# The first expert slot fed from ten early tiles and two late ones, the last projection and the first head in halves

## The chip, the cores and the metric

The kernel runs on one core of a Trainium2 chip, in one launch. The metric is device time in microseconds (us), and lower is better. Every run of the kernel before lies between 775.5 and 778.18 us, with 776.9 us in the middle of three.

## The reference

Three stages follow each other. Only the shapes and the steps that the change touches are kept here.

```python
# 1 attention: B=2, H=8, S=768, D=64
q_bits = (q @ proj > 0); k_bits = (k @ proj > 0)      # proj: 64 x 6
mask = bucket(q_bits)[:, None] == bucket(k_bits)[None, :]
attn = softmax(where(mask, q @ k.T / 8, -1e9)); attn_out = attn @ v
x = attn_out -> (1536, 512)
# 2 gated layer, 512 -> 1536 -> 512
xn = x / sqrt(mean(x*x) + 1e-6) * rms_g
x = (silu(xn @ w_gate) * (xn @ w_val)) @ w_out
# 3 eight experts, each token goes to one
e_idx = argmax(x @ gate_w); weight = softmax(x @ gate_w)[e_idx] * sigmoid(x @ out_gate)[e_idx]
for e in range(8):
    rows = x[e_idx == e]
    out[e_idx == e] = weight * (relu(rows @ w1[e]) @ w2[e])      # 512 -> 1024 -> 512
```

## The kernel before

There are five engines: PE (matrix products), ACT, DVE and POOL (elementwise work) and SP (which only starts transfers). Each follows its own hand-written list and waits on semaphores. Nearly every product is made of three, from operands split into a high and a low part (names that end in `_h` and `_l`), so an operand is first converted (high, mostly ACT) and then subtracted (low, mostly DVE).

**Attention** takes the 16 heads in 8 pairs. A pair is a `period` of 12 steps. A step makes one score tile of 128 queries by 768 keys on PE (`scores`), its row maximum on DVE (`maxes`, L1442) and its exponential on ACT (`exps`, L1199). After three steps DVE inverts the sums (`denoms`, L1452 and L1454), POOL multiplies the three tiles by them (L710) and PE turns the tiles (`turn`, L899), five steps behind the scores. Pair 0 has no predecessor that prepares it. Its keys and queries come in eight transfers (`load_first` on SP and L1278 on ACT), ACT converts them (`first_highs`, L1173; `own_queries`, L1177), DVE makes the low parts of its first head (L1571) and POOL those of its second head (`second_lows`, L614), and PE projects both heads onto the six directions in halves of the sequence, numbered `m` = 0 to 3 (`project_first`, L865). PE passes the first microseconds with 36 products whose results nobody reads (`keep_warm`, L977), and makes two further groups of eight of them in period 0.

**The gated layer** makes all 12 tiles (128 tokens each) of the hidden values and then, tile after tile, `project(tt)` on PE: 36 products of 512 columns into a bank of PSUM (L1086). ACT scales the result into `x2` (L1320). PE turns `x2` and multiplies it with the router's weights (`turn_x2`, L1068; `gate_logits`, L1076), DVE chooses the expert (`choose`, L1673 to L1683), PE counts the token's place among those of its expert (`ranks`, L1059), DVE makes the row number `dest` (`put`, L1688 to L1696), and POOL scatters the 128 rows of the tile to the DRAM tensor `routed`, which is ordered by expert (L821). In PE's list the routing of tile `tt` stands between the products of the next two tiles.

**The experts** are eight slots, each up to 256 rows. A slot needs its rows (`rows_in`), turned on PE (`turn_rows`, L1120), in high and low part (`rowsT`, L1349; `low_rowsT`, L1745), and the expert's weights, which come in four pieces of 1 MB (`load_piece`) and are split by ACT and DVE (`split_piece`, L1338 and L1626). Then `up` makes 96 products of 256 columns (L1134), ACT and DVE split the hidden values (L1354, L1751), and `down` makes two halves of 24 products of 512 columns (L1146). The rows of the next slot are loaded and turned meanwhile. The first slot has nobody before it: SP waits until all twelve scatters have landed (L579) and only then loads `rows_in[0]`. PE makes 36 idle products between the count and `turn_rows(0)`, and ten more between that and `up`.

```python
sp.wait_ge(scattered, 16 * NT)                                         # L579
sp.dma_start(rows_in[0][:], blocks_v[:, first_block(0)]).then_inc(rows_loaded[0], 16)
```

Of the kernel before, what the change touches and what calls it, by code (L numbers as in the profile page):

```python
# [11 lines left out]
I32 = mybir.dt.int32  # L12
# [10 lines left out]
FIRST_PROJ_STEP = 5  # L23

# [8 lines left out]
def build(nc, q, k, v, proj, w_gate, w_val, w_out, rms_g, router, out_gate, w1, w2, out):  # L33
# [46 lines left out]
    with ExitStack() as ctx:  # L80
# [27 lines left out]
        logits = at("logits", [P128, NT, 2 * E], F32)  # L108
# [19 lines left out]
        dest_f = at("dest_f", [P128, NT], F32)  # L128
        dest = at("dest", [P128, NT], I32)
        count_f = at("count_f", [1, E], F32)  # L130
# [93 lines left out]
        DVE_LOWS = ([(1, c) for c in range(C)] + [(tg, c) for tg in (2, 3) for c in range(C)])  # L224
        addr[0] = x2_offset
# [29 lines left out]
        for i in range(3):  # L255
# [17 lines left out]
                 "alone_put exp_done denom_done rden_ready norm_done turned high_ready low_ready pv_done "  # L273
# [3 lines left out]
                 "x2_turned x2T_made logits_made logits_out best_made flag_made before_made z_made route_step route_exp ranks_made counted placed "  # L277
                 "table_made scattered w1_high w2_high w1_low w2_low rows_turned rowsT_high rowsT_low hid_made "
# [5 lines left out]
         alone_put, exp_done, denom_done, rden_ready, norm_done, turned, high_ready, low_ready, pv_done,  # L284
# [3 lines left out]
         x2_turned, x2T_made, logits_made, logits_out, best_made, flag_made, before_made, z_made, route_step, route_exp,  # L288
         ranks_made, counted, placed,
         table_made, scattered, w1_high, w2_high, w1_low, w2_low, rows_turned, rowsT_high, rowsT_low, hid_made,  # L290
# [13 lines left out]
        rows_loaded = [sem(f"rows_loaded{i}") for i in range(2)]  # L304
        rows_stored = [sem(f"rows_stored{i}") for i in range(2)]
# [65 lines left out]
        row_banks = (ps_t[0], ps_o)  # L371
        out_banks = (ps_t[1], ps_p)
# [55 lines left out]
        def _(sp):  # L428
# [53 lines left out]
            def load_first(r, halves):  # L482
                for w, src in ((KEYS, k_v), (QUERIES, q_v)):
                    for half in halves:
                        sp.dma_start(first_raw[lanes(half), w, r], src[0, r]).then_inc(first_in[2 * r + w], 16)

            load_first(0, (0,))
            load_first(1, (0, 1))
# [10 lines left out]
            sp.wait_ge(cleared, 6)  # L499
# [88 lines left out]
        def _(pool):  # L588
# [178 lines left out]
            for n, rows in enumerate((k_b[0], k_b[1], q_b[1])):  # L767
                for r in range(2):
                    wait(pool, cleared, 2 * n + r)
                    nc.gpsimd.memset(rows[lanes(1 - r), r].bitcast(F32), 0.0).then_inc(cleared, 1)  # L770
# [1040 lines left out]
```

## Time and profile before

| | us |
|---|---|
| median of three runs | 776.9 |
| the profiled run, as timed | 776.07 |
| its span, first to last instruction | 774.3 |
| PE busy within the span | 754.2 |
| attention, to about | 245 |
| gated layer: hidden values, to about | 450 |
| gated layer: projection and routing, to about | 565 |
| from the last projection to the first expert product | 565.4 to 581.3 |
| eight slots | 581.3 to 769 |

The profile is one execution. Its clock starts at the first instruction. Where PE is busy without a break its work is the time, whatever the others do. Where PE stands, the view of waits names what it stood for, and the chain of waits shows, backwards from the last instruction, which step released which. The time as timed is 1.8 us above the span; that part lies around the kernel.

### The profile page before, as it was taken

How to read it: one execution, taken by the hardware profiler on the slowest of the kernel's cores; microseconds unless marked ns; L12 is line 12 of the kernel's file. 1: busy time of each engine (PE TensorE's matmuls, PEld its weight loads, DVE VectorE, ACT ScalarE, POOL GpSimd, SP SyncE). 2: the span in 40 equal slices, each digit the busy share in tenths (PEclk: the TensorE clock that was granted, in tenths of full speed). 3: DMA queues.
4: the chain of work that ended last, by engine and by line, in shares of the span. 5: the costliest groups of instructions: out<-in, count | busy, mean ns of one | idle time of the engine just before them, and what ended most of it. 6: DMA issues, size and time to landing. Idle time of an engine off the chain costs nothing.

```text
span 774.3 us, 13374 instructions
## 1 busy us (share of the span) xinstructions
PE 754.2 (97%) x4562; PEld 688.4 (89%) x4562; DVE 476.7 (62%) x930; ACT 377.1 (49%) x671; POOL 313.0 (40%) x345
## 2 busy tenths in 40 slices
PE   7999999999999999999999999999979999999996
PEld 6789899888888999999999988888869998899995
DVE  6999999999987654334334344455554554565430
ACT  5888889888887311111111133534333444455431
POOL 7977877789788573333443001211210011000111
PEclk9999999999999999999999999999999999999999
DMA  7897679659501222111110040022352656765400
GB/s 205 216 271 212 191 202 231 191 137 239 133 10 44 78 76 63 41 41 41 41 52 29 0 164 25 21 84 76 137 184 87 229 193 223 254 217 197 157 25 23
DMA packets 54011, 97.53 MB, mean 126 GB/s; under 512 B 6761, under 2 KB 21109, under 8 KB 53960
## 3 DMA queue, kind: packets, MB, share of 16 engines
q1 hardware_dynamic: 49496, 86.48, 38.1%
q0 software_dynamic: 2240, 6.31, 2.1%
q10 hardware_dynamic: 2224, 4.08, 1.9%
q8 instruction: 30, 0.49, 0.3%
q14 instruction: 21, 0.17, 0.1%
HBM read 58.25 MB, written 22.10 MB: 104 GB/s over the span
## 4 chain that ended last, share of the span: by engine, by line
PE 83%; DVE 9%; issue 3%; ACT 2%; DMA 2%; POOL 1%; ACTq 0%; POOLq 0%; DVEq 0%
PE ps_t L1086 13%; PE ps_s L946 13%; PE ps_s L1134 12%; PE ps_t L946 6%; PE ps_t L899 6%; PE ps_t L1146 6%; PE ps_p L1146 6%; DVE pT_l L1460 4%; PE ps_o L946 3%; PE ps_p L946 3%; PE ps_s L885 3%; DVE negmax L1442 3%; PE ps_s L886 3%; PE ps_o L914 1%; PE ps_o L916 1%
## 5 line engine op out<-in xcount | busy, mean ns | idle before, releaser
L710 POOL TENSOR_SCALAR probs<-probs,rden,alone 128x768 f32<-128x768 f32 x96 | 93.9, 992 | 33.8 <-DVE rden L1454 33.7
L1460 DVE TENSOR_TENSOR pT_l<-ps_t,pT_h 128x384 fp32r<-128x384 f32 x192 | 97.6, 549 | 5.8 <-ACT pT_h L1209 4.7
L946 PE MATMUL ps_s<-xn,w_h 128*128 128x384 f32 x384 | 97.5, 334 | 0.0
L1199 ACT ACTIVATE probs<-ps_s,negmax 128x768 f32<-128x768 f32 x96 | 87.2, 908 | 17.5 <-DVE negmax L1442 16.9
L1209 ACT ACTIVATE pT_h<-ps_t 128x384 fp32r<-128x384 f32 x192 | 85.4, 492 | 16.6 <-PE ps_t L899 15.3
L1442 DVE TENSOR_REDUCE negmax<-ps_s 128x1 f32<-128x770 f32 x96 | 91.0, 948 | 4.0 <-PE ps_s L886 3.1
L1134 PE MATMUL ps_s<-rowsT_h,expert_w 128*128 128x256 f32 x512 | 92.4, 281 | 0.6 <-DVE rowsT_l L1745 0.6
L899 PE MATMUL ps_t<-ident,probs 128*128 128x128 f32 x576 | 87.4, 282 | 4.6 <-DVE pT_l L1460 2.7
L827 POOL DMA_INDIRECT out_dram<-rows_out,rows_in x16 | 15.8, 986 | 182.2 <-ACT rows_out L1360 182.2
L899 PEld LDWEIGHTS ps_t<-ident,probs 128*128 128x128 f32 x576 | 63.0, 140 | 24.4 <-DVE pT_l L1460 10.2
L1626 DVE TENSOR_TENSOR expert_w<-piece,expert_w 128x2048 fp32r<-128x2048 f32 x32 | 72.6, 2291 | 15.4 <-ACT expert_w L1338 15.1
L1134 PEld LDWEIGHTS ps_s<-rowsT_h,expert_w 128*128 128x128 f32 x512 | 79.1, 189 | 1.1 <-issue 0.8
L821 POOL DMA_INDIRECT routed<-x,dest x12 | 21.1, 1758 | 128.2 <-DVE x L1695 128.2
L1134 PE MATMUL ps_s<-rowsT_l,expert_w 128*128 128x256 f32 x256 | 71.9, 281 | 0.0
L946 PEld LDWEIGHTS ps_s<-xn,w_h 128*128 128x128 f32 x384 | 69.4, 188 | 0.0
L885 PE MATMUL ps_s<-k_a,q_a 128*128 128x384 f32 x192 | 65.1, 339 | 1.9 <-ACT probs L1199 1.0
L1751 DVE SCALAR_TENSOR_TENSOR hidT_l<-ps_s,hidT_h 128x512 fp32r<-128x512 f32 x32 | 22.1, 689 | 71.3 <-ACT hidT_h L1354 71.3
L886 PE MATMUL ps_s<-k_b,q_b 128*128 128x384 f32 x192 | 64.8, 337 | 0.0
L946 PE MATMUL ps_s<-xn,w_l 128*128 128x384 f32 x192 | 64.1, 334 | 0.0
L1338 ACT ACTIVATE expert_w<-piece 128x2048 fp32r<-128x2048 f32 x32 | 60.2, 1908 | 0.0
L1086 PE MATMUL ps_t<-wo_h,hs_h 128*128 128x512 f32 x144 | 59.2, 411 | 0.0
L1086 PE MATMUL ps_t<-wo_h,hs_l 128*128 128x512 f32 x144 | 56.4, 392 | 0.0
(243 smaller groups left out, 1695.5 us busy)
## 6 DMA issues: line engine op xcount, KB each, us to landing
piece<-in_moe_w_dram SPq DMA_DIRECT2D x32, 1024.0 KB, 6.3
routed<-filler SPq DMA_DIRECT2D x56, 257.0 KB, 4.6
k_a<-qk_h SPq DMA_DIRECT2D x28, 192.0 KB
rows_in<-routed ACTq DMA_DIRECT2D x7, 514.0 KB, 3.7
rawv<-in_v_dram SPq DMA_DIRECT2D x8, 384.0 KB, 5.9
w_raw<-in_moe_w_gate_dram SPq DMA_DIRECT2D x12, 256.0 KB, 3.1
w_raw<-in_moe_w_val_dram SPq DMA_DIRECT2D x12, 256.0 KB, 3.4
wo_raw<-in_moe_w_out_dram SPq DMA_DIRECT2D x12, 256.0 KB, 2.6
```

Source lines behind the costliest of these rows:

```text
L710: nc.gpsimd.tensor_scalar(pr, pr, rden[:, j:j + 1], alone[:, j:j + 1], ALU.mult, ALU.add).then_inc(norm_done, 1)
L885: nc.tensor.matmul(o, q_a[par][:, r, queries], k_a[par][:, r, keys], start=True, stop=False)
L886: mm = nc.tensor.matmul(o, q_b[par][:, r, queries], k_b[par][:, r, keys], start=False, stop=True)
L899: mm = nc.tensor.transpose(ps_t[kt % 2][:, i * P128:(i + 1) * P128], probs[:, 3 * g + i, kt * P128:(kt + 1) * P128], ident[:])
L946: mm = nc.tensor.matmul(unit_banks[tg][w][:, 0:G], a_[par][:, w, c, :], xn_at(tg, part, c), start=(n == 0), stop=(n == 3 * C - 1))
L1086: mm = nc.tensor.matmul(ps_t[par][:], a_[par][:, f, :], b_[:, f, :], start=(f == 0 and n == 0), stop=(f == NF - 1 and n == 2))
L1134: mm = nc.tensor.matmul(hid_banks[b][:, i * ROWS:(i + 1) * ROWS], a_[:, side, c, f:f + P128], b_[:, c, :], start=(n == 0), stop=(n == 3 * ...
L1146: mm = nc.tensor.matmul(out_banks[half][:], a_[:, c, half_cols(half)], b_[:, side, c, :], start=(c == 0 and t == 0), stop=(c == CF - 1 and ...
L1199: nc.scalar.activation(probs[:, j].rearrange("p (a n) -> p a n", a=2), third(ps_s[j % 2]), ACT.Exp, bias=negmax[:, j:j + 1], accum_out=psu ...
L1209: nc.scalar.activation(pT_h[u % 4][:], ps_t[kt % 2][:, 0:G], ACT.Copy).then_inc(high_ready, 1)
L1442: nc.vector.tensor_reduce(negmax[:, c], with_floor(ps_s[j % 2]), AX.XY, ALU.max, negate=True).then_inc(max_done, 1)
L1460: nc.vector.tensor_tensor(pT_l[u % 4][:], ps_t[kt % 2][:, 0:G], pT_h[u % 4][:].bitcast(F32), ALU.subtract).then_inc(low_ready, 1)
```

## The change

It has three parts and some waits that belong to them.

**The hand-over to the first slot.** SP loads the 512 data columns of `rows_in[0]` after ten scatters (`early_rows_in`). The last two columns of each row (the output row and the factor) are loaded once all twelve have landed. The scatter of tile 10 waits for the early load. PE multiplies the early rows with the unit matrix into two cleared banks (`turn_early`, eight products) instead of turning them. The rows of tiles 10 and 11 are added to these banks by 16 products of 256 columns: the tile's high and low part times a matrix of ones and zeros (`onehot`), which has a one where a token goes to a place among the first 256 (`add_late`). `up` of every slot now takes the eight products with the high rows first and the four with the low rows after them. The 58 idle products around the hand-over are gone.

**The last projection in halves.** `project(11)` is made for the left 256 columns and then for the right ones, with the router's work for the left half between them. `ranks(tt-1)` moves to the end of `project(tt)`. `choose` reads PSUM directly.

**The first head in halves.** The transfers of pair 0 are in another order. The low part of the first head's queries is made in two halves, and the fourth projection (`m` = 3) comes behind the first scores. Four clears move from POOL to DVE and five small writes of `proj_w` from DVE to POOL. ACT normalises the third tile of pair 0 and makes `own_queries(1)` later, the first `denoms` stands ahead of the fourth `maxes`, and the two groups of eight idle products become groups of four. DVE's `denoms` and POOL's `put_alone` of all later periods wait for `first_norm`, too.

```diff
 sp.wait_ge(first_in[KEYS], 32)          # new, between the loads of head 0 and of head 1
...
-            sp.wait_ge(scattered, 16 * NT)
-            sp.dma_start(rows_in[0][:], blocks_v[:, first_block(0)]).then_inc(rows_loaded[0], 16)
+            sp.wait_ge(scattered, 16 * (NT - LATE))
+            sp.dma_start(rows_in[0][:, :, 0:DM], blocks_v[:, first_block(0), :, 0:DM]).then_inc(early_rows_in, 16)
+            sp.wait_ge(late_scattered, 16 * LATE)
+            sp.dma_start(rows_in[0][:, :, DM:DM + 2], blocks_v[:, first_block(0), :, DM:DM + 2],
+                         allow_slow_non_contiguous=True).then_inc(rows_loaded[0], 16)
...
+                if tt == NT - LATE:
+                    pool.wait_ge(early_rows_in, 16)
...
             for tt in range(NT):
                 project(tt)
+            project(NT - 1, 1)
+            def turn_early(first, last):
+                pe.wait_ge(early_rows_in, 16)
+                pe.wait_ge(banks_cleared, 1)
+                for n in range(first, last):
+                    c, half = divmod(n, 2)
+                    nc.tensor.matmul(place_in_first(c)[:, half_cols(half)], rows_in[0][:, half, c * P128:(c + 1) * P128],
+                                     ident[:], start=(half == 0 and c % 2 == 0), stop=False)
+            def add_late(i):
+                pe.wait_ge(onehot_made, i + 1)
+                pe.wait_ge(late_low, (1, 3)[i])
+                for c in range(C):
+                    for part in (late_h, late_l):
+                        mm = nc.tensor.matmul(place_in_first(c), part[i][:, c * P128:(c + 1) * P128], onehot[i][:],
+                                              start=False, stop=(i == LATE - 1 and c % 2 == 1 and part is late_l))
...
-                step(nc.vector.tensor_reduce(one(dest_f, tt), chosen[:], AX.X, ALU.add))
-                nc.vector.tensor_copy(one(dest, tt), one(dest_f, tt))
+                    step(nc.vector.tensor_reduce(one(dest_f, i), chosen[:], AX.X, ALU.max))
+                    nc.vector.tensor_scalar(onehot[i][:], slot_f[:], one(dest_f, i), None,
+                                            ALU.is_equal).then_inc(onehot_made, 1)
...
+                        if j == 2:
+                            own_queries(1)
+                        if j == 3:
+                            act.wait_ge(rden_ready, 1)
+                            act.wait_ge(alone_put, 1)
+                            nc.scalar.activation(probs[:, 2], probs[:, 2], ACT.Identity, bias=alone[:, 2:3],
+                                                 scale=rden[:, 2:3]).then_inc(first_norm, 1)
-                        if j in (0, 2, 3):
-                            high_ahead(1, 1, max(0, j - 1))
+                        if j in (0, 3, 4):
+                            high_ahead(1, 1, max(0, j - 2))
...
                 wait(dve, norm_done, 3 * (n - 4))
+                if not (isinstance(P, int) and P == 0):
+                    dve.wait_ge(first_norm, 1)
```

PE's list before, from the end of the last projection to the first expert product. `x_174` is `x2`, `ps_o` the bank for turned tiles, `ps_p` that of the router, and the products `ps_t<-ident` and `ps_s<-ident` with no second operand are the idle ones.

```order
L1076 MATMUL ps_p<-gates,x2T_178 128x16 [waits logits_out,x2T_made]
L1076 MATMUL ps_p<-gates,x2T_178 128x16 x3
L977 MATMUL ps_s<-ident 128x128 x6
L1059 MATMUL ps_s<-flag_b,before_b 128x8 [waits flag_made]
L1060 MATMUL ps_s<-before_tile_b,ones_b 128x8
L977 MATMUL ps_s<-ident 128x128 x6
L1112 MATMUL ps_s<-before_tile_b,ones_b 128x8 [waits before_made]
L1113 MATMUL ps_s<-neg_base_b,ones_b 128x8
L977 MATMUL ps_s<-ident 128x128 x36
L1120 MATMUL ps_t<-ident,rows_in_180 128x128 [waits rows_loaded0]
L1120 MATMUL ps_t<-ident,rows_in_180 128x128 x3
```

The same place after the change:

```order
L1130 MATMUL ps_p<-gates,x2T_188 128x16 [waits x2T_left,z_made]
L1130 MATMUL ps_p<-gates,x2T_188 128x16
L1112 MATMUL ps_o<-ident,x_184 128x128 [waits x2_made,x2T_made]
L1112 MATMUL ps_o<-ident,x_184 128x128
L1177 MATMUL ps_t<-ident,rows_in_190 128x128 [waits banks_cleared,early_rows_in]
L1177 MATMUL ps_t<-ident,rows_in_190 128x128
L1130 MATMUL ps_p<-gates,x2T_188 128x16 [waits x2T_made,z_made]
L1130 MATMUL ps_p<-gates,x2T_188 128x16
...
L1103 MATMUL ps_s<-flag_b,before_b 128x8 [waits flag_made]
...
L1185 MATMUL ps_t<-onehot_179,late_h_176 128x256 [waits late_low,onehot_made]
```

The idle products have gone, two of the four router products stand ahead of the right half's turning, and the load of the early rows is waited for in front of the other two.

ACT's list before, from the start to the first turned tile of pair 0 (`k_a`, `q_b` and `q_a` are the operands of the scores, `qk_h` and `raw` belong to the next pair, `pT_h` is the turned tile):

```order
L1173 ACTIVATE k_a_103<-first_raw,lane_scale 128x768 [waits first_in2]
L1173 ACTIVATE q_b_106<-first_raw,lane_scale 128x768 [waits first_in3]
L1177 ACTIVATE q_a_105<-first_raw 64x768
L1199 ACTIVATE probs,psums<-ps_s,negmax 128x768 [waits max_done]
L1189 ACTIVATE qk_h_100<-raw_112 128x768 [waits qk_in1]
L1199 ACTIVATE probs,psums<-ps_s,negmax 128x768 [waits max_done] x2
L1189 ACTIVATE qk_h_100<-raw_112 128x768
L1199 ACTIVATE probs,psums<-ps_s,negmax 128x768 [waits max_done]
L1189 ACTIVATE raw_112<-raw_112 128x768
L1199 ACTIVATE probs,psums<-ps_s,negmax 128x768 [waits max_done]
L1209 ACTIVATE pT_h_119<-ps_t 128x384 [waits turned]
```

And after:

```order
L1264 ACTIVATE k_a_103<-first_raw,lane_scale 128x768 [waits first_in2]
L1264 ACTIVATE q_b_106<-first_raw,lane_scale 128x768 [waits first_in3]
L1290 ACTIVATE probs,psums<-ps_s,negmax 128x768 [waits max_done]
L1280 ACTIVATE qk_h_100<-raw_112 128x768 [waits qk_in1]
L1290 ACTIVATE probs,psums<-ps_s,negmax 128x768 [waits max_done] x2
L1268 ACTIVATE q_a_105<-first_raw 64x768
L1290 ACTIVATE probs,psums<-ps_s,negmax 128x768 [waits max_done]
L1364 ACTIVATE probs<-probs,alone,rden 128x768 [waits alone_put,rden_ready]
L1280 ACTIVATE qk_h_100<-raw_112 128x768
L1290 ACTIVATE probs,psums<-ps_s,negmax 128x768 [waits max_done]
L1280 ACTIVATE raw_112<-raw_112 128x768
L1300 ACTIVATE pT_h_119<-ps_t 128x384 [waits turned]
```

One conversion (`q_a`) has moved behind three exponentials, and one instruction on `probs` has come in; both stand in front of the first `pT_h`.

## Rows read from the trace of the kernel before

**Rows 1.** Chain of waits, 562 to 600 us: start, us, what.

```profile
562.51 2.89 PE ps_t L1086 x12
...
565.42 0.70 ACT x L1320
...
567.50 1.08 PE ps_p L1076 x8
...
568.61 0.19 DVE logits L1673
...
570.31 0.17 DVE dest_f L1690
...
571.90 2.84 DMA routed<-x,dest
...
574.75 3.73 DMA rows_in<-routed
...
581.29 11.50 PE ps_s L1134 x96
```

**Rows 2.** Chain of waits, the first 24 us.

```profile
2.71 5.92 DMA first_raw<-in_q_dram
...
14.39 1.00 ACT probs L1199 x2
...
19.93 2.94 POOL probs L710 x3
...
22.91 0.87 PE ps_t L899 x6
```

**Rows 3.** Timeline, 545 to 582 us, SP and POOL: start, us, what.

```profile
550.16 10.80 SPq L555 DMA_DIRECT2D piece<-in_moe_w_dram  x3
...
558.92 2.48 POOL L821 DMA_INDIRECT routed<-x,dest  x1 [7.95 <-DVE x L1695]
```

**Rows 4.** Windows: length, busy (count) by engine, clock, DMA share, GB/s.

```profile
565.00:566.00 1.00, 0.43 (x4) 0.12 (x2) 0.47 (x4) 0.58 (x1) 0.00 (x0) 1.00 1.04 410
566.00:567.00 1.00, 0.66 (x4) 0.42 (x4) 0.52 (x5) 0.26 (x2) 0.00 (x0) 1.00 0.20 80
```

**Rows 5.** Groups of ACT and DVE, 540 to 582 us: busy us, mean ns.

```profile
L1320 ACT ACTIVATE x<-ps_t,rinv 128x512 f32<-128x512 f32 x3 | 2.1, 691 | 3.5 <-PE ps_t L1086 3.5
L1349 ACT ACTIVATE rowsT_h<-ps_t 128x512 fp32r<-128x512 f32 x1 | 0.6, 598 | 5.3 <-PE ps_t L1120 5.3
...
L1745 DVE TENSOR_TENSOR rowsT_l<-ps_t,rowsT_h 128x512 fp32r<-128x512 f32 x1 | 0.7, 692 | 3.1 <-ACT rowsT_h L1349 3.1
```

**Rows 6.** Windows around the hand-over, columns as above.

```profile
566.00:570.00 4.00, 2.61 (x21) 2.14 (x22) 1.74 (x13) 1.10 (x4) 0.96 (x1) 1.00 0.23 89
570.00:573.30 3.30, 3.30 (x19) 2.95 (x18) 2.26 (x10) 3.18 (x3) 0.96 (x1) 0.50 0.00 0
...
576.60:580.00 3.40, 1.47 (x13) 1.47 (x14) 0.27 (x2) 0.78 (x2) 0.00 (x0) 1.00 1.03 377
```

**Rows 7.** Timeline, the first 25 us: start, us, what, idle before.

```profile
1.32 0.48 DVE L1536 MEMSET proj_w<- 128x512 f32 x1
1.60 6.67 PE L977 MATMUL ps_t<-ident 128*128 128x128 f32 x36 [1.60 <-POOL ident L748]
...
12.01 0.84 ACT L1177 ACTIVATE q_a<-first_raw 64x768 fp32r<-64x768 f32 x1
...
20.27 0.84 ACT L1189 ACTIVATE raw<-raw 128x768 f32<-128x768 f32 x1
...
23.49 0.88 ACT L1209 ACTIVATE pT_h<-ps_t 128x384 fp32r<-128x384 f32 x2 [1.08 <-PE ps_t L899]
```

**Rows 8.** Timeline at 160 us on DVE, and its piece in the chain.

```profile
160.47 0.94 DVE L1442 TENSOR_REDUCE negmax<-ps_s 128x1 f32<-128x770 f32 x1
161.33 0.15 DVE L1452 TENSOR_SCALAR denom<-psums 128x3 f32<-128x3 f32 x1
...
160.70 0.63 issue
```

More of the change, by code:

```diff
@@ L480, in fill, with load_first @@
                     sp.dma_start(routed_v[:, first + t], filler[:]).then_inc(fill_done, 16)
[L482 to L488, printed above, removed]
+            def load_first(r, w, half):
+                sp.dma_start(first_raw[lanes(half), w, r], (k_v, q_v)[w][0, r]).then_inc(first_in[2 * r + w], 16)
+            load_first(0, KEYS, 0)
+            load_first(0, KEYS, 1)
+            load_first(0, QUERIES, 0)
+            sp.wait_ge(first_in[KEYS], 32)
+            for w in (KEYS, QUERIES):
+                for half in range(2):
+                    load_first(1, w, half)
             load_qk(1, 1)
@@ L749, in _ @@
                                     pattern=[[-1, P128]], channel_multiplier=1).then_inc(ident_ready, 1)
+            pool.wait_ge(ident_ready, 1)
+            for r in range(2):
+                wait(pool, cleared, r)
+                nc.gpsimd.memset(k_b[0][lanes(1 - r), r].bitcast(F32), 0.0).then_inc(cleared, 1)
+            pool.wait_ge(cleared, 2)
             nc.gpsimd.memset(ones_f[:], 1.0)
@@ L1016, in _ @@
             pe.wait_ge(cleared, 2)
-            for m in range(4):
+            for m in range(3):
                 project_first(0, m)
@@ L1064, in turn_x2 @@
                     pe.wait_ge(silu_step, 2 * TG * NF)
+                wait(pe, x2T_made, tt)
                 wait(pe, x2_made, tt + 1)
-                wait(pe, x2T_made, tt)
-                for c in range(C):
+                for c in range(C // 2 if tt == NT - 1 else 0, C):
                     tr = nc.tensor.transpose(ps_o[:, c * P128:(c + 1) * P128],
@@ L1281, in _ @@
             act.wait_ge(scales_ready, 1)
-            for r in range(2):
-                for w in (KEYS, QUERIES):
-                    first_highs(w, r)
-                own_queries(r)
+            first_highs(KEYS, 0)
+            first_highs(QUERIES, 0)
+            own_queries(0)
+            first_highs(KEYS, 1)
+            first_highs(QUERIES, 1)
             period(0, 0, before=False)
@@ L1450, in denoms @@
                 wait(dve, norm_done, 3 * (n - 4))
+                if not (isinstance(P, int) and P == 0):
+                    dve.wait_ge(first_norm, 1)
                 wait(dve, exp_done, 3 * n)
@@ L1496, in period @@
                 for j in range(PAIR_STEPS):
+                    if isinstance(P, int) and P == 0 and j == 3:
+                        denoms(0, 0)
                     if s:
                         maxes(P, j)
-                    if s and j > 0 and j % 3 == 0:
+                    if s and j > 0 and j % 3 == 0 and not (isinstance(P, int) and P == 0 and j == 3):
                         denoms(P, j // 3 - 1)
@@ L1536, in _ @@
             nc.vector.memset(proj_w[:].bitcast(F32), 0.0).then_inc(prefilled, 1)
+            for rows in (k_b[1], q_b[1]):
+                for r in range(2):
+                    op = nc.vector.memset(rows[lanes(1 - r), r].bitcast(F32), 0.0)
+            op.then_inc(prefilled, 1)
             dve.wait_ge(prefilled, 1)
@@ L1683, in choose @@
                 nc.vector.tensor_reduce(one(z, tt), own_gate[:], AX.X, ALU.add).then_inc(z_made, 1)
+                wait(dve, route_exp, 2 * tt + 1)
+                nc.vector.tensor_scalar(one(esum, tt), one(esum, tt), 1e-9, None, ALU.add)
             def put(tt):
```

304 lines of the change are left out of this document (218 added, 86 removed).

## The prediction, made before the changed kernel ran

> **What bounds the kernel now.** I read the busy times first. PE is busy in 754.2 of the 774.3 us of the span, so apart from its own work only about 20 us can be won, and the view of PE's gaps says where they lie. The chain of waits around the hand-over from the projection to the experts comes next [rows 1]: the last product of the projection ends at 565.4, the first expert product starts at 581.3. Between them PE is needed only for short steps. The reader should see the two transfers there, 2.84 us for the last scatter and 3.73 us for the load of the rows behind it, and that they follow each other and the routing of the last tile. The second place is the start [rows 2]: the transfer of the queries (5.92 us), the first exponential at 14.39, three normalisations on POOL (2.94 us), and the first turned tile at 22.91. From 24 us to 565 us and from 581 us to 768 us PE has no gap of note, so a step made earlier in those stretches brings nothing.
>
> **Part 1, the last projection in halves.** One product of 512 columns takes 2.89 / 12 = 0.24 us with the drain of the last one, about 0.23 without, one of 256 columns 11.50 / 96 = 0.12 [rows 1]. The 72 half products take 8.6 us where 36 took 8.3, 0.3 more, and turning the left half inside them adds two short instructions (about 0.13 each, as 1.08 us for eight). The projection so ends at about 566.0 instead of 565.4. `ranks` only changes its place. This cost lies on the path.
>
> **Part 2, the early load.** Ten scatters must have landed. That of tile 9 starts at 558.92 before [rows 3], because `ranks(9)` stands in the second sixth of the next projection; at the end of its own it comes some 1.5 us sooner. With 2.5 us on POOL and 2.8 us to land, five if the queues are full, it is done at 562 to 564. SP has by then issued the last of its three 1 MB pieces (it ends with that at 550.16 + 10.80 = 561.0 [rows 3]), and their bytes move until 566: 410 GB/s in the microsecond before, 80 in the one after [rows 4]. The half megabyte of rows goes through the same queue and comes to 567.3 if it stands behind the piece (1.3 us at 400 GB/s), to 566.2 if it doesn't. PE asks for it at about 566.9. I take 0.4 us of waiting on the path; the bounds are 0 and 1.5. The two columns that follow and the scatters of tiles 10 and 11 have until 589, when the first result is scaled. The pieces behind them on SP's queue are not wanted before slot 1's first hidden values, more than 20 us later. The load for slot 1 on ACT now waits for both late scatters; these land near 575, and it is issued near 578. These costs are zero under that cover; without it each microsecond of delay would count once.
>
> **Part 3, from the last product to `up`.** The right half goes through these steps, from the rows of whole tiles: ACT scales 256 columns (0.69 for 512 [rows 5], so 0.45), PE turns two chunks (0.4), ACT copies them (0.60 for 512 [rows 5], so 0.4), PE makes the second half of the router's products (half of 1.08 [rows 1]: 0.5). DVE needed 570.31 + 0.17 - 568.61 = 1.87 us to the row number [rows 1]; it loses the first copy (0.19), gains a small addition (0.17) and the comparison that makes the ones and zeros (256 columns, against 0.69 for 512 [rows 5]: 0.35), together 2.2. Four late products give the first bank (0.5), and ACT's copy of it (0.6) lets `up` begin. That is 5.05 us and seven hand-overs of about 0.05, 5.4 in all. PE's own work meanwhile, six products with the unit matrix as two instructions each (12 x 0.13 = 1.6) and eight of tile 10 (1.0), fits beside DVE's 2.2 us but for some 0.3 that I leave in the range. A full-precision product of 128 moving columns is not in this trace; from the 16-column ones (0.13) up to 0.24 each it costs 0 to 1.3 us more. I take the low end, since the turning instructions with 128 columns have the same pace as those with 16.
>
> `up` therefore starts at 566.0 + 5.4 + 0.4 = 571.8. Its first group still waits for the other bank's copy and low part, 1.3 us after the first copy, against 0.96 us of products that can go ahead: 0.4 us. As if it began at 572.2, against 581.3, it gains 9.1 us; I round to **9.0**, from 7.4 to 9.8. The regrouped products of the other slots cost nothing, since every one keeps its own weight load and its column count.
>
> **PE's clock at the hand-over.** Before, the granted clock is 1.00 (2.4 GHz) while PE is busy 2.61 of 4.00 us (566 to 570), falls to 0.50 (1.2 GHz) at 570.0 and is back after 3.3 us, in which only products that nobody reads ran; and it does not fall behind 576.6 to 580, where PE was busy 1.47 of 3.40 us [rows 6]. The change takes the fillers away and puts its work into the time of the first fall. The Trainium skill (TensorE: Matmul & The Clock Gate, What's actually happening) calls the lower clock the default, which activity lifts, and so speaks against taking away fillers; the first fall in the rows agrees, the second stretch does not. By the rule `up` would begin at the half clock. From the rows alone the price is this: 3.3 us at 1.2 GHz with PE busy for 2.6 to 3.3 of them costs 1.3 to 1.6 us.
>
> **Part 4, the start.** The order of the first loads brings keys and queries of head 0 to ACT about 1 to 2 us sooner, since head 1 no longer shares the queues; but PE's idle products last until 1.60 + 6.67 = 8.3 [rows 7], and DVE has four clears more, 0.48 x 768 / 512 = 0.7 us each [rows 7], ahead of the direction matrices. The first exponential comes at 12.3 to 13.4 instead of 14.4. What follows is ACT's list. Before the first `pT_h` at 23.49 it has five exponentials and three conversions, 5 x 0.95 + 3 x 0.84 = 7.3 us, in 9.1 us. After the change it has `own_queries(1)` (0.84 [rows 7]) and the normalisation (0.9) more, 9.05 us, and still waits 0.9 to 1.1 us for maxima. So `pT_h` starts at 12.3 + 9.05 + 0.9 = 22.3 at best and at 13.4 + 9.05 + 1.1 = 23.6 at worst. PE's turning comes 1.5 to 3 us sooner because POOL has one tile less (2.94 / 3 = 1.0), but what is late next is ACT. The gain is -0.1 to 1.2; I take **0.7**, as head 0's transfers are certainly relieved.
>
> **Part 5, the waits for `first_norm`.** 28 `denoms` on DVE and 28 on POOL wait for a semaphore that was set long before. DVE is behind them with `maxes` and low parts, for which ACT and PE wait. Their price is that of one waiting instruction. The timeline has the maximum until 160.47 + 0.94 = 161.41 and `denom` from 161.33 on, so the two waits that stand there now are hidden under the maximum, although the chain books 0.63 us there without a cause [rows 8]. I take 0, at most 28 x 0.03 = 0.8.
>
> **Sum.** 9.0 + 0.7 + 0 = 9.7 us. The profiled run took 776.07 us (span 774.3 and 1.8 around it), which gives 766.4. The median of the runs is 0.8 above the profiled one, and that is what will be compared: 776.9 - 9.7 = **767.2**.
>
> **Rivals.**
> - *The clock falls during the hand-over or under the first `up`.* For it: the first fall [rows 6], and 58 fillers less. Against: the second stretch, which was emptier and did no harm, and that real work fills 566 to 571. 767.2 + 1.5 = 768.7.
> - *The hand-over is late by another step.* Either the early rows land near 568.5 instead of 567.3, or DVE, which has to get through tile 10's row number, one copy and three conversions or low parts (2.8 us and hand-overs, from 564.1 to 567.3) before `choose(11)`, falls behind. Against: it has some 0.3 us of slack. 767.2 + 1.4 = 768.6.
> - *The start gives nothing,* as ACT's list has no room: 767.9.
> - *Slower than before.* The 28 waits on DVE cost real time. It decides from 9.7 / 28 = 0.35 us each. If each cost as much as the whole unexplained piece again (0.63 [rows 8]), it would be 17.6 us, and 776.9 - 9.7 + 17.6 = 784.8. Against: the neighbouring waits are hidden, and PE, not DVE, bounds most of attention.
> - *The change does not do what it says:* the early load is held until all scatters are done anyway. The list of SP waits for ten only, so I give it next to nothing; only the 3.73 us would come back, 770.9.
>
> **Chances.** Forecast 0.52, clock 0.22, late step 0.12, start 0.10, slower 0.02, early load held 0.02. The range runs from 764.9 (0.8 more at the hand-over, 0.5 more at the start, and 1.0 if the compared runs lie as low as the profiled one) to 770.2 (clock and late step together). A measurement of this kernel can tell about 0.3% (2.3 us) from no change. All cases but the waits lie below 774.6, so faster has 0.97, the same 0.01, slower 0.02.
>
> **What would show it.** In the profile after: the last product of the projection at 565 to 566.5 (after the start's shift, 0.7 less), `up` 5.5 to 6.5 us behind it instead of 15.9, no transfer in the chain between them but perhaps the early rows, the first `pT_h` at 22.3 to 23.6, the periods of attention at their old 7.03 us for three steps, and the clock in the 5 us around the first `up`. I would be wrong if the chain shows the early rows for over 1.5 us, if the half clock lasts for more than one such stretch, or if PE waits for DVE's `denoms`.

## The result, and the profile after

The changed kernel takes 770.75 us (median of 5 runs, 768.67 to 772.21) against 777.05 (775.5 to 778.18) before: a ratio of 0.9912, 95% interval 0.9891 to 0.9933, so it is faster, clear of noise. The forecast was 767.2 (764.9 to 770.2), so of 9.7 us of gain 6.3 came. Two of the five runs (768.67 and 768.88) lie inside the range, and the median does not; these two have the higher mean clock of PE (0.999 against 0.994 to 0.997). The profiled run took 770.92 us with a span of 769.1; in spans the gain is 774.3 - 769.1 = 5.2 us, because the profiled run of before was one of its faster ones. From ACT's scaling of the last part to the first product of the experts it now takes 575.61 - 566.23 = 9.4 us, where before needed 15.9 and the forecast had 5.8.

The chain of waits of after, 554 to 588 us (start, us, what), answers to [rows 1]:

```profile
554.25 2.20 DVE expert_w L1768
...
557.82 4.93 DMA routed<-x,dest
...
562.77 6.36 DMA rows_in<-routed
...
569.17 0.71 PE ps_t L1177 x4
569.88 0.37 PE ps_p L1130 x4
570.25 1.05 PE ps_t L1177 x4
571.30 0.85 PE ps_s L1177 x4
...
572.18 1.06 PE ps_s L1177 x4
573.24 0.65 PE ps_t L1185 x4
...
574.87 0.60 ACT first_rowsT_h L1466
```

Before the change the chain ran through the last projection and the last tile's routing. Now it leaves PE at 552.9 us, with the flag of tile 9, and goes through a low part of expert 0 on DVE (2.20), scatter 9 (L861) and the load of the early rows (L602); only from 569.17 on is PE in it again. (The low part stands on DVE between tile 9's flag and its row number, so it holds the scatter up; no run moved it.) Two of the products with the unit matrix (unit products from here on; four instructions, `x4`) take 1.05 us here, which is twice the 0.13 an instruction that the forecast had. PE's timeline gives the length of the gap and the first product of the experts (start, us, engine, line, idle before):

```profile
569.17 0.71 PE L1177 MATMUL ps_t<-ident,rows_in 128*128 128x128 f32 x4 [1.91 <-DMA rows_in<-routed]
...
575.61 1.19 PE L1225 MATMUL ps_s<-first_rowsT_h,expert_w 128*128 128x256 f32 x8 [0.25 <-ACT first_rowsT_h L1466]
```

The windows of after around the hand-over answer to [rows 6] (length, busy of PE, PE's weight loads, DVE, ACT, POOL, then granted clock, DMA share, GB/s):

```profile
566.00:569.20 3.20, 1.04 (x9) 0.73 (x7) 0.92 (x3) 0.86 (x2) 0.00 (x0) 1.00 0.43 168
...
571.00:573.00 2.00, 2.00 (x13) 1.94 (x11) 1.29 (x8) 0.48 (x3) 0.00 (x0) 0.50 0.34 132
...
567.00:568.00 1.00, 0.26 (x2) 0.02 (x1) 0.46 (x2) 0.38 (x1) 0.00 (x0) 1.00 0.33 127
568.00:569.00 1.00, 0.00 (x0) 0.00 (x0) 0.00 (x0) 0.00 (x0) 0.00 (x0) 1.00 0.07 29
```

PE is busy 1.04 of the 3.20 us to 569.2, and from 570.1 to 573.5 the clock is 0.50 (1.2 GHz). Six of the eight unit products and `ranks` of the last tile lie in that stretch. So both of the faults that the forecast had as rivals are there at once: the rows are late and the clock is down. What SP issued, against [rows 3]:

```profile
549.89 11.17 SPq L577 DMA_DIRECT2D piece<-in_moe_w_dram  x3
562.77 0.37 SPq L602 DMA_DIRECT2D rows_in<-routed  x1
```

The third 1 MB piece was issued by 549.89 + 11.17 = 561.06, and the rows stand right behind it.

### The profile page after: what moved, and what is told of

The parts are those of the page before. It is cut to its first block, busy times and chain, and to the rows that moved or that the text cites. A ratio compares the mean times of both kernels' runs of the same rounds, so it can differ in the third digit from the quotient of the medians.

```text
span 769.1 us, 13409 instructions
## 1 busy us (share of the span) xinstructions
PE 751.1 (98%) x4556; PEld 687.1 (89%) x4556; DVE 477.9 (62%) x930; ACT 377.9 (49%) x675; POOL 300.3 (39%) x346
## 4 chain that ended last, share of the span: by engine, by line
PE 83%; DVE 10%; issue 3%; ACT 2%; DMA 1%; POOL 0%; POOLq 0%; DVEq 0%; ACTq 0%
PE ps_s L988 13%; PE ps_t L1146 12%; PE ps_s L1225 8%; PE ps_t L988 7%; PE ps_t L941 6%; PE ps_p L1240 6%; PE ps_t L1240 6%; PE ps_s L1230 4%; DVE pT_l L1593 4%; PE ps_o L988 3%; PE ps_p L988 3%; DVE negmax L1573 3%; PE ps_s L926 2%; PE ps_s L927 2%; PE ps_o L956 1%
## 5 line engine op out<-in xcount | busy, mean ns | idle before, releaser
L861 POOL DMA_INDIRECT routed<-x,dest x12 | 11.8, 981 | 139.7 <-DVE x L1850 102.7
L1225 PE MATMUL ps_s<-rowsT_h,expert_w 128*128 128x256 f32 x448 | 62.3, 281 | 0.0
L1225 PEld LDWEIGHTS ps_s<-rowsT_h,expert_w 128*128 128x128 f32 x448 | 57.6, 189 | 0.6
L1146 PE MATMUL ps_t<-wo_h,hs_h 128*128 128x512 f32 (+1 forms) x144 | 58.0, 403 | 0.0
L1146 PE MATMUL ps_t<-wo_h,hs_l 128*128 128x512 f32 (+1 forms) x144 | 55.2, 383 | 0.0
L1146 PE MATMUL ps_t<-wo_l,hs_h 128*128 128x512 f32 (+1 forms) x144 | 54.9, 381 | 0.0
```

Source lines behind the costliest of these rows:

```text
L1146: mm = nc.tensor.matmul(bank, a_[par][:, f, :], b_[:, f, cols], start=(f == 0 and n == 0), stop=(f == NF - 1 and n == 2))
L1225: nc.tensor.matmul(hid_banks[b][:, i * ROWS:(i + 1) * ROWS], a_[:, side, c, f:f + P128], high[:, c, :], start=(c == 0 and t == 0), stop=False)
```

## The experiments

All absolute times are medians of 4 to 12 runs. The experiments were measured on four chips, on which the kernel before had medians of 777.88 (hand-over alone, start alone, both pieces behind, products in the gap), 778.41 (router's products first, first two unit products moved, queries sooner, `ranks` back), 776.59 (one piece behind, all unit products in waits, longer cover) and 777.67 us (old start in the covered kernel). So a difference of 1 us between two medians from different chips shows nothing. Across chips I go by the ratios to the kernel before and by places in the traces. The start of the first projection product ("the mark", 450.21 before, 449.97 after) takes the start of the kernel out of a comparison; these are its lines in the chains of before and of after:

```profile
450.21 5.94 PE ps_t L1086 x26
```

```profile
449.97 6.16 PE ps_t L1146 x27
```

### Why the early rows were late

**Both pieces behind the rows.**

```diff
             load_piece(0, 3)
-            load_piece(1, 2)
-            load_piece(1, 3)
             sp.wait_ge(scattered, 16 * (NT - LATE))
             sp.dma_start(rows_in[0][:, :, 0:DM], blocks_v[:, first_block(0), :, 0:DM]).then_inc(early_rows_in, 16)
+            load_piece(1, 2)
+            load_piece(1, 3)
```

> The change, with the two w2 pieces of slot 1 issued behind the early rows instead of ahead of them. Theory 'the rows are late because SP and the transfers are busy with pieces': scatter 9 lands in 3 us instead of 4.93, the rows in under 4 us instead of 6.36, at 565 or earlier; PE does not wait for them (1.91 us before), the first up product comes at 573.7 to 574, the time is 1.5 to 1.9 us below the full change: 769. If the gap was also what brought the clock down, all products run at full clock and another 1.5 us go: 767.4. Rival 'the rows need 6 us in any case, for their half megabyte': less than 0.7 us.

Measured: 767.43 us (766.89 to 768.32), ratio 0.9865, 0.9851 to 0.988. Its queues, and its chain from the end of the projection:

```profile
560.51 0.37 SPq L600 DMA_DIRECT2D rows_in<-routed  x1
...
557.59 0.96 POOL L861 DMA_INDIRECT routed<-x,dest  x1 [9.33 <-DVE x L1850]
...
rows_in<-routed SPq DMA_DIRECT2D x1, 512.0 KB, 3.9
```

```profile
566.00 0.48 ACT x L1419
...
567.03 0.45 PE ps_t L1177 x4
...
569.23 0.18 PE ps_s L1103
...
569.43 0.58 PE ps_s L1177 x4
570.01 0.48 PE ps_t L1185 x4
570.49 0.48 PE ps_s L1185 x4
570.97 0.49 PE ps_t L1185 x4
...
571.48 0.61 ACT first_rowsT_h L1466
```

Scatter 9 starts at 557.59 and SP issues the rows behind it at 560.51, 2.9 us later instead of 4.95; the rows (last column, us from issue to landing) take 3.9 instead of 6.36. The gap on PE is gone, and the clock stays at 1.00:

```profile
566.00:570.00 4.00, 3.58 (x30) 3.16 (x30) 2.32 (x14) 1.46 (x5) 0.96 (x1) 1.00 1.04 377
```

ACT's copy starts 3.39 us sooner than in after, of which 449.97 - 449.76 = 0.21 is the start: 3.18 us from this one move. The rival, rows that need 6 us by themselves, is out.

**Only the last piece behind the rows.**

```diff
             load_piece(1, 2)
-            load_piece(1, 3)
             sp.wait_ge(scattered, 16 * (NT - LATE))
             sp.dma_start(rows_in[0][:, :, 0:DM], blocks_v[:, first_block(0), :, 0:DM]).then_inc(early_rows_in, 16)
+            load_piece(1, 3)
```

> The change, with only the last piece (1 MB, issued at 560.7 to 561.1) behind the early rows, and the one issued at 556.4 where it was. Theory 'the rows' 6.36 us come from the piece that is ahead of them in the queue': scatter 9 still takes 4 to 5 us and lands at 562.5, but the rows land 3.7 to 4 us after their issue, at 566.2 to 566.5, before PE asks; no gap on PE, clock 1.00, time as with both pieces behind, 767.5. Rival 'the late scatter is the other half of it': rows at 567.5 to 568, PE waits 0.5 to 1 us, 768 to 769.

Measured: 767.34 us (767.01 to 767.58). The rows are issued 4.66 us after scatter 9 starts (557.07), as slow as in after, and land 3.9 us later, at about 565.6:

```profile
561.73 0.37 SPq L601 DMA_DIRECT2D rows_in<-routed  x1
...
rows_in<-routed SPq DMA_DIRECT2D x1, 512.0 KB, 3.9
```

The other profiles agree. From the start of scatter 9 to the issue of the rows it takes 4.7 to 5.1 us in the five with a piece under way and 2.9 to 3.4 in the seven without. The rows take 6.0 to 6.6 us in the four with a piece directly ahead of them and 3.7 to 4.1 in the eight without. So the piece that is under way when scatter 9 starts costs it 1.3 to 2.2 us, the one directly ahead of the rows costs them 1.9 to 2.9, and moving the second alone is enough, since PE asks at 566.5.

### Why the clock fell, and what it cost

**Products that nobody reads in the gap.**

```diff
+            keep_warm(ps_t[1][:, 3 * P128:4 * P128], 14)
             turn_early(0, 2)
             gate_logits(NT - 1, range(C // 2, C))
```

> The change, with 14 products that nobody reads (0.13 us each) where PE waits for the early rows, 567.3 to 569.2. Theory 'the clock falls because PE stood idle there': the granted clock stays at 1.00 from 570 to 573.5, the unit products run at 0.13 us each instead of 0.26, first up product at 574.1 instead of 575.6, time 769.3. Rival 'the fall has another cause, as before the change, where it fell at 570 as well with PE busy 2.6 of 4.0 us': clock 0.50 again, time unchanged at 770.8. If a product with the unit matrix and two instructions costs 0.26 each at the full clock too, they keep that length with the clock at 1.00.

Measured: 768.85 us (768.61 to 769.13), ratio 0.9881, 0.9867 to 0.9896. The rows are as late as in after (6.40 us), and yet:

```profile
562.34 6.40 DMA rows_in<-routed
...
571.09 0.58 PE ps_s L1177 x4
...
573.14 0.60 ACT first_rowsT_h L1467
```

```profile
571.00:572.00 1.00, 1.00 (x11) 1.00 (x10) 0.93 (x7) 0.20 (x1) 0.00 (x0) 1.00 0.67 263
```

The clock stays up (1.00), and the four instructions take 0.58 us instead of 1.05. Counted from the mark (449.52), ACT's copy comes at 123.62 instead of 124.90: the clock cost 1.28 us, at the lower end of the 1.3 to 1.6 that the forecast took from the rows. It also goes with the scatter of the time: after has mean clocks of 0.994 to 0.997 in its three slower runs (770.75 to 772.21) and 0.999 in the other two (768.67 and 768.88). These two are as fast as the kernel with the gap filled. The groups lie at least 1.9 us apart, more than 1.28; only one of these runs has a profile, so the rest is not explained.

**The router's products ahead of the unit products.**

```diff
             turn_x2(NT - 1)
-            turn_early(0, 2)
             gate_logits(NT - 1, range(C // 2, C))
+            turn_early(0, 2)
```

> The change, with the first two unit products behind the right half of the router's products instead of ahead of them; the early rows stay late (569.1). Theory 'the wait for the rows costs 1.9 us because the router's products and DVE's whole chain stand behind it on PE': the right half runs at 567.8, the flag is there at 569.2, the eight unit products start when the rows land and then bound PE. With the clock at 0.50 from about 570: 569.2 + 8 x 0.5 + 1.0 + 1.0 = 574.6 to 575.0 for the first up, time 769.8; with the clock at 1.00: 572.9, 768.1. Rival 'what counts is the work behind the landing, in whatever order': no gain over the full change, 770.8.

Measured: 769.86 us (768.47 to 770.24). The rows land at 568.9, the clock is 0.50 from about 568.3 to 571.7, and the unit products follow in a row:

```profile
568.87 2.07 PE ps_t L1177 x8
570.94 0.85 PE ps_s L1177 x4
...
573.86 0.60 ACT first_rowsT_h L1466
```

From the mark (449.47) the copy comes at 124.39, 0.51 us sooner than in after. The first `up` product comes at 574.60 and the median is where the first theory had them, but half of that 1.0 us is the earlier start of this run (its mark is at 449.47 against 449.97). With the flag made meanwhile, PE's own work behind the landing (unit products at the half clock) took over as the bound. The order was worth 0.5, not 1.9.

### PE's own list behind the flag

**Two unit products ahead of the turning** (on top of both pieces behind the rows):

```diff
-            turn_x2(NT - 1)
             turn_early(0, 2)
+            turn_x2(NT - 1)
```

> As the kernel with the pieces behind the rows, and the first two unit products ahead of the right half's turning, where PE waits 0.5 us for ACT's scaling and the rows are already there. Theory 'behind ranks(11) PE's own list bounds the hand-over (0.6 of unit products, 1.0 of tile 10, 1.0 of tile 11, against 1.0 for DVE's ones and zeros)': the list behind ranks gets no shorter by this move, only the stretch in front, so up comes 0.1 us sooner, and the time stays at 767.3. Rival 'any unit product moved into a wait comes off the path whole': 0.5 us, 766.9.

Measured: 767.65 us (767.39 to 768.11). Two other kernels with the same order as without the move had 767.34 and 767.82 on this chip, so no gain shows. Then **all of them in waits that PE has anyway:**

```diff
-            turn_x2(NT - 1)
             turn_early(0, 2)
+            turn_x2(NT - 1)
+            turn_early(2, 4)
             gate_logits(NT - 1, range(C // 2, C))
-            turn_early(2, 6)
+            turn_early(4, 8)
             ranks(NT - 1)
-            turn_early(6, 8)
```

> As the kernel with the pieces behind the rows, with all eight unit products in waits that PE has anyway: two ahead of the right half's turning, two ahead of the right half's router products, four ahead of ranks(11); none is left behind ranks. Theory 'behind ranks(11) PE's own list bounds the hand-over': there 0.58 + 0.96 + 0.98 us became 0.96 + 0.98, first up product 0.5 us sooner, time 766.9 to 767.0 where that kernel has 767.4 to 767.5. Rival 'the flag or the ones and zeros bound it': under 0.15 us, as when only two were moved.

Measured: 766.98 us (766.65 to 767.24). Its chain behind the flag:

```profile
568.87 0.18 PE ps_s L1103
...
569.07 0.60 PE ps_t L1185 x4
569.68 0.48 PE ps_s L1185 x4
570.15 0.58 PE ps_t L1185 x4
570.76 0.61 ACT first_rowsT_h L1466
```

From `ranks` to ACT's copy it takes 1.89 us, where both pieces behind the rows alone have 571.48 - 569.23 = 2.25. So 0.36 of PE's 0.58 us were on the path, and the front of the hand-over grew by 0.1. Moving two that already lay in a wait brought nothing; moving the two behind the flag brought 0.26 in these traces. The medians alone do not show it: on the same chip the kernel with one piece behind the rows, whose list is otherwise the same, has 767.34, and the two ranges overlap (766.65 to 767.24, 767.01 to 767.58).

**A longer cover for the low part** (on top of that): the high products of the second bank's first block stand ahead of the first low products.

```diff
-                        for c in range(C):
...
+                        if not (s_ == 0 and b == 1 and i == 0):
+                            high_part(b, i)
+                        if s_ == 0 and b == i == 0:
+                            high_part(1, 0)
```

> As the kernel with all unit products in waits, and in slot 0 the high products of the second bank's first block stand ahead of the first low products, so that PE has 1.92 instead of 0.96 us of work before it asks for the low part. Theory 'the stall of 0.26 us in the first group costs itself and 0.26 us of a fresh start': both go, another 0.5 us, 766.4. Rival 'the weights' low parts or DVE's second low part is late next': the stall comes back behind 1.92 us and the gain is under 0.2.

Measured: 766.85 us (766.34 to 767.31), ratio 0.9871, 0.9854 to 0.9887. In the chain the stall is gone:

```profile
572.33 2.14 PE ps_s L1223 x16
574.47 0.48 PE ps_s L1237 x4
```

From ACT's copy to the first `down` it takes 584.06 - 571.59 = 12.47 us; the kernel above has 583.55 - 570.76 = 12.79. That is 0.32 and not 0.5, and in the medians 0.1, within their spread. All kernels with the rows in time and the new start have ratios of 0.9855 to 0.988 with overlapping intervals, 2.5 to 4.4 us below the change as it was made (0.9912); the times do not say which of them is the fastest.

### The start, and the projection

**The hand-over alone**, with the start's edits taken back, of which these are two of the places:

```diff
-            first_highs(KEYS, 0)
-            first_highs(QUERIES, 0)
-            own_queries(0)
-            first_highs(KEYS, 1)
-            first_highs(QUERIES, 1)
+            for r in range(2):
+                for w in (KEYS, QUERIES):
+                    first_highs(w, r)
+                own_queries(r)
...
-                if not (isinstance(P, int) and P == 0):
-                    dve.wait_ge(first_norm, 1)
```

> The change without its start (loads, clears, normalisation and first_norm waits as before). The trace of after has the start's gain at 0.24 us at 450 us (first projection product at 449.97 against 450.21) and at nothing at 529.75 us, while 0.7 us was in the forecast. Theory 'the start is worth nothing behind the projection': within 0.3 us of the full change, so about 770.8, first up product at 575.6 to 575.9. Rival 'the start is worth its 0.7 us, and something else lost it': 771.4 or more.

Measured: 770.99 us (770.45 to 772.78), ratio 0.9912, as the full change, but the first `up` product at 577.03 and not at 575.6 to 575.9. Its clock was 0.50 for twice as long as in after:

```profile
568.90:575.70 6.80, 6.45 (x31) 6.39 (x32) 2.32 (x16) 0.60 (x3) 1.64 (x2) 0.51 0.10 39
```

**The start alone**, the same edits on the kernel before:

> The start alone, with the old hand-over. By the theory that the start is worth nothing: 776.8 to 777.1, with 0.2 us won at 47 to 450 us and the hand-over as in before (15.9 us from the last product of the projection to the first up). By the forecast's term: 776.3. If it and the hand-over alone do not add up to the full change, the two parts hinder each other.

Measured: 776.75 us (775.57 to 778.65; one of twelve runs took 2619.6 us and is left out, with it the median is 776.96), ratio 0.999, 0.9979 to 1.0002. Neither run could settle 0.5 us against falls of the clock worth 1.3. So I took the start back **in the kernel whose clock stays up** (the covered one):

> As the kernel with all unit products in waits and the covered first group (766.85, runs 766.34 to 767.31), but with the start as before the change; with the clock at 1.00 through the hand-over a difference in the start is not hidden by the clock's falls. By the starts of the first projection product (449.3 to 450.1 with the new start, 449.7 in the mean of nine; 450.21 and 450.28 with the old one) the new start is worth 0.5 us: first projection product at 450.2, time 767.4. By the forecast's term: 0.7, 767.6. By the rival that it gives nothing, and by the full change against the hand-over alone (both 0.9912): 766.9.

Measured: 768.07 us (767.52 to 768.37), no run below 767.5, where the new start has 766.34 to 767.31. These are 1.2 us, but from two chips on which the kernel before differs by 1.1 as well (777.67 and 776.59). By the ratios, 0.9878 (0.9862 to 0.9895) against 0.9871 (0.9854 to 0.9887), it is 0.5 us, and the intervals overlap. The marks scatter by 0.9 us from run to run:

| Start of the kernel | Mark, us, one profiled run each | Mean |
|---|---|---|
| old | 450.21, 450.28, 451.13 | 450.54 |
| new | 449.97, 449.75, 449.76, 449.52, 449.47, 449.58, 450.14, 449.69, 449.28, 449.24, 450.13 | 449.68 |

Every old mark is later than every new one, which speaks for a gain. How large it is stays open: the marks give 0.24 us in the pair first compared, 0.6 on the chip that has one old mark (450.28) and three new ones (449.75, 449.76, 449.52), 0.86 over all, and the ratio of the start alone 0.8, with no gain still inside its interval. The third old mark has no partner on its chip. The expectation that the start gives nothing is unlikely but not refuted by the times.

One late mark has a cause that its trace shows. In the profile of the covered kernel (450.13) the clock was down in the start as well:

```profile
19.40:22.90 3.50, 3.50 (x14) 2.96 (x13) 2.04 (x3) 3.36 (x6) 2.55 (x4) 0.51 0.96 224
```

PE had waited 1.34 us up to 16.93 and 0.81 up to 18.67. No other profile here has this. The new start halves the two groups of idle products that stand next to these waits; whether that lets the clock fall was not tested.

**Head 1's queries scaled sooner** (on top of both pieces behind the rows):

```diff
-                        if j == 2:
+                        if j == 1:
                             own_queries(1)
```

> As the kernel with the pieces behind the rows, and ACT scales head 1's own queries behind the second exponential instead of behind the third; it waits 1.0 us for a maximum there. Theory 'ACT's list bounds the start and this work can lie in ACT's wait': PE's gap of 1.92 us at 18.7 goes, pT_h starts at 22.5 instead of 23.3, and 0.5 to 0.8 us of it are left at 450 us: 766.7. Rival 'DVE's maxima bound it by then, or POOL's two normalisations': less than 0.2 us.

Measured: 767.82 us (767.37 to 768.35), no gain. PE's gap at 18.7 is gone, but `pT_h` starts at 23.65 and not sooner. The chain shows the rival: the fourth exponential waits for DVE, whose `denom` stands ahead of the fourth maximum and waits for the third exponential.

```profile
17.06 1.00 ACT probs L1290 x2
...
18.09 0.18 DVE denom L1585
...
18.50 0.97 DVE negmax L1573
```

**`ranks` at its old place** (on top of both pieces behind the rows):

```diff
-                    if f == NF - 1 and 1 <= tt < NT - 1:
-                        ranks(tt - 1)
+                    if f == 1 and tt >= 2 and not part:
+                        ranks(tt - 2)
```

> As the kernel with the pieces behind the rows (767.4 in its call), and ranks of tiles 0 to 9 again between the second and third sixth of the next-but-one projection, as before the change. Theory 'the place behind the last product of a projection costs 0.03 us a tile' (from 450 to 529.5 us the kernels with the new place need 79.75 to 79.78 us, those with the old one 79.53 and 79.54): the last projection ends 0.35 us sooner and the time falls by 0.3 to 0.4. Scatter 9 starts about 1 us later and the rows land at 565 instead of 564, still ahead of PE's demand. Rival 'the later scatter takes it back': the rows become the end of the chain again, no gain or a loss.

Measured: 767.34 us (767.14 to 767.68), no difference. The turning of tile 7 starts 79.30 us after the mark (528.88 - 449.58); with the new place it is 79.32 to 79.34, in the kernel before and with the start alone 79.10 and 79.09. So the projections did become some 0.03 us a tile slower, and the place of `ranks` is not the reason. The twelve products behind the turning take 2.77 us where they took 2.75, in the chains of before and of after; which edit does this stays open.

## Why the prediction was wrong

The median lies 0.55 us above the range. Two steps failed together: the early rows landed at 569.13 and not at 567.3, because their load was priced by its bytes alone, and PE's clock, taken to stay up, fell behind the wait that this made. The steps behind the last projection were 0.8 us too short as well. I count in the profiled pair, from the mark or from the chain, against the terms of the sum.

- **Part 1, the halves: 1.05 us, not 0.6.** From the mark ACT's scaling of the last part starts at 566.23 - 449.97 = 116.26, before at 565.42 - 450.21 = 115.21. The halves account for the forecast's 0.6 or a little more; the rest, 0.2 to 0.3, is the 0.03 us a tile (0.24 by tile 7), which no term had.
- **Part 2, the early load: 1.9 us of waiting, not 0.4.** This step failed, beyond its upper bound of 1.5, which the forecast had also named as a sign of being wrong. The forecast had scatter 9 land at 562 to 564 and it did, at 562.75. But it took 1.3 us for the rows behind the piece, their bytes at 400 GB/s, and the bytes were indeed nearly through at 567.3: the transfers carry 127 GB/s from 567 to 568 and 29 from 568 to 569. The landing came 1.8 us behind that. The load of before shows the same: 3.73 us [rows 1] for bytes worth 1.3, so some 2.4 us of a load are not bytes, and the forecast left them out. With them it would have had the landing at about 566 + 3.73 = 569.7 and the failure before the run. That the piece ahead makes the rest is shown by the runs with one and with both pieces behind the rows (3.9 us from issue).
- **PE's clock: 1.28 us, forecast at 0.** The price in the rival was right; its chance of 22% was not. I had set the emptier stretch at 576.6 [rows 6] against it, and real work from 566 to 571. That work was then not there, since the late rows left PE idle: the two faults were treated as apart and are one. With the rows in time or the gap filled the clock did not fall at the hand-over in any of the nine profiles of such kernels; where PE waited for late rows it fell in all three. The Trainium skill (TensorE: Matmul & The Clock Gate, What's actually happening) says that the lower clock is the default and that activity lifts it, which speaks against taking the fillers away. The trace agrees (1.91 us of idleness, then 0.50 from 570.1 to 573.5).
- **Part 3, the steps to `up`: 6.2 us, not 5.4,** with rows in time and the clock up (566.00 to 572.22 in the run with both pieces behind). The single steps hold: scaling 0.48 (0.45), flag 0.98 behind the logits, copy 0.61. Unit products at full clock take 0.58 / 4 = 0.145 us an instruction (0.13). What was mis-sized is the sentence that PE's own work fits beside DVE's 2.2 us "but for some 0.3": behind the flag stood 1.54 us of it, of which the run with all of them in waits took back 0.36. The steps in front of DVE were 0.25 longer than the forecast's 1.95 (566.00 to 568.20).
- **The stall in the first group: 0.53 us, not 0.4.** In the run with both pieces behind, PE idles 0.26 us, and its first low product is longer by as much (0.74 for four against 0.48).
- **Part 4, the start: 0.24 in this pair, 0.24 to 0.9 by all marks.** The 0.7 is neither shown nor refuted. The first exponential came at 13.13 and `pT_h` at 23.32, inside the forecast (12.3 to 13.4, 22.3 to 23.6), and ACT's list runs without a pause up to it from 19.17 on, but what released that stretch is DVE's fourth maximum. Nor does the gain pass through the first `pT_h` alone: the hand-over alone, with the old start, has it at 23.27 and still a later mark.
- **Part 5, the waits for `first_norm`: nothing,** as forecast. The turning of head pairs has the same period, 54.39 - 47.36 = 7.03 us (54.40 - 47.38 = 7.02 before), and from there to the mark it takes 449.97 - 47.36 = 402.61 us (402.83 before). The rival on the slower side is out.

The sum of the differences in the profiled pair: 1.5 (rows) + 1.25 (clock) + 0.8 (steps) + 0.45 (projection) + 0.1 (stall) + 0.5 (start) = 4.6, and 9.7 - 4.6 = 5.1, against 5.2 in the spans. In the medians before stands 0.98 us above its profiled run and after 0.17 below its own: 5.15 + 0.98 + 0.17 = 6.3. The range ended at 770.2, clock and late step together; it left no room for the steps and the projection beside them.

## What to carry to other kernels

A load that is moved earlier starts behind whatever its queue and the engines of the transfers have just been given, so price it as the bytes ahead of it plus the full time, issue to landing, of a load of its size, never as bytes alone (here 569.7 by that sum, 569.13 measured), and put large pieces that are not wanted yet behind it. PE pays for a wait a second time if the wait brings its clock down: count a wait and the fall behind it as one case, and work that fits into the wait, useful or not, is worth placing there. When a wait is taken off the path, add up what is left on the engine's own list behind the last release; here it bound at once.

## What the runs showed of the hardware

- The same scatter, counted from its start to the issue of the load that waits for it, took 2.9 to 3.4 us with no piece under way and 4.7 to 5.1 with one; half a megabyte of rows took 3.7 to 4.1 us from its issue, and 6.0 to 6.6 behind 1 MB on the same queue.
- In after the clock fell 0.9 us after the idleness had ended, when PE was fully busy again, and stayed at 1.2 GHz for 3.4 us. In the profile of the hand-over alone it fell while PE still waited and was there for 6.8 us, with PE busy in all but the first 0.5.
- A subtraction of 64x384 on DVE took 0.56 us alone and 1.41 beside two of POOL's; DVE and POOL of after, and then of the kernel with the covered first group:

```profile
8.24 0.56 DVE L1709 TENSOR_TENSOR q_a<-first_raw,q_b 64x384 fp32r<-64x384 f32 x1
...
10.70 1.41 DVE L1709 TENSOR_TENSOR q_a<-first_raw,q_b 64x384 fp32r<-64x384 f32 x1
...
10.69 2.29 POOL L639 TENSOR_TENSOR k_b<-first_raw,k_a 64x384 fp32r<-64x384 f32 x2 [0.88 <-ACT k_a L1264]
```

```profile
10.70 0.56 DVE L1716 TENSOR_TENSOR q_a<-first_raw,q_b 64x384 fp32r<-64x384 f32 x1
...
10.81 2.47 POOL L639 TENSOR_TENSOR k_b<-first_raw,k_a 64x384 fp32r<-64x384 f32 x2 [1.00 <-ACT k_a L1271]
```

In five profiles POOL's pair started 0.01 to 0.18 us ahead of DVE's subtraction. In each of them DVE's ended 1.42 or 1.43 us after POOL's start, whatever the lead (in after 10.70 + 1.41 - 10.69), and DVE paid 0.7 to 0.9 us. In four DVE was ahead by 0.04 to 0.15 us, took 0.56, and POOL's pair took 2.44 to 2.54 us instead of 2.3. In two POOL was ahead by 0.84 and 0.86 us, and neither paid. So the later one waits, until some 0.86 us after POOL's start in the first case; that is read from eleven profiles, and nothing here was made to prove it. It is one source of the start's scatter.
